# Attention and two gated layers on one core: SyncE asks for a batch's loads in another order

## Chip, core and metric

The kernel runs on one core of one Trainium2 chip. The metric is the device time of one execution in microseconds.

## What is computed

Eight batches of 8 heads, 576 positions and head size 64; all arithmetic is float32, and the large products are done in three float32r products each (high x high, high x low, low x high).

```python
def sm_attn(qq, kk, vv):
    s = scale * np.matmul(qq, kk.transpose(0, 1, 3, 2))
    a = np.exp(s - np.max(s, axis=-1, keepdims=True))
    a = a / (np.sum(a, axis=-1, keepdims=True) + 1e-09)
    return np.matmul(a, vv)
p_packed = sm_attn(p, k, v)                # 32 packed rows per head
x = sm_attn(q, p_packed, p_packed)         # -> 4608 tokens x 512
xn = x / rms(x) * rms_g
g = xn @ w_gate                            # 512 x 1536
y = (silu(g) * (xn @ w_val)) @ w_out       # 1536 x 512
h = ((y @ w1) * (y @ w2)) @ w3             # 512 x 1024, then 1024 x 1024
out = h @ w_out2                           # 1024 x 512
```

## The kernel before

**Stages.** (1) A fused product, `wf = w3 @ w_out2`, in eight row blocks (`fuse`, L668 to L670), with the attention of batch 0 threaded between its pieces. It ends 65 us into the span. (2) Eight batches of 24 slots each, some 88 us a batch. (3) The last layer, from about 770 us to the end, which the change does not touch.

**A slot.** Slot n (f = n // 2 within the batch, t = n % 2) computes 128 rows of gate and value for 288 tokens on TensorE (`into`, L688 to L690). ScalarE takes tanh (L1005), VectorE makes g_s and g_h (L1240, L1246), ScalarE casts the high half of g_hx (L1012), VectorE subtracts to get the low half (L1260). Two slots fill one g_hx tile k = n // 2 (there are two such tiles). From slot 2 on TensorE also does half of the output product of tile n // 2 - 1 (`outof`, L708 to L710), 512 of the 576 tokens. The other 64 tokens of a tile go to memory with a 64 KB store, `rest_scratch<-g_hx`, which ScalarE issues in the even slots for the tile before (L986); the stores count up two semaphores in turn, and the cast in an odd slot waits until the store of the tile two before has landed, since it overwrites that tile.

**Attention between the slots.** After some slots an item of the next batch's attention runs on TensorE (the table `SLOT_ITEM`): M (a piece of the folded input weights, L652, six pieces per batch), S1 (scores of keys, L603), AT (L608), PV (values, L615), PT, S2 (scores of queries, L626), Z (L636), SS (L640). M(b,2) and M(b,3) are in slots 1 and 2, AT of the next batch in 3 and 4, PV in 5, PT in 6, S2 in 7 and 10, Z in 11 and 14, M(b,4) and M(b,5) in 12 and 13, SS in 16, M(b+1,0) and M(b+1,1) in 18 and 20, S1 of batch b+2 in 22 and 23. Batch 0's attention and S1(1,0) run inside the fused product, S1(1,1) after slot 0.

**Loads.** SyncE issues nearly all transfers in one order, written by hand, and stands still at each semaphore wait in it. The loads: `load_kp(a)` packed queries and keys of batch a (L342, L343), waits for S1 of batch a - 1; `load_v(a)` values (L350), waits for PV(a - 1); `load_q(a, t)` half of the queries (L357), waits for S2(a - 1, t); `load_w_in(a, part)` a 1 MB piece of w_gate or w_val (L366, two buffers), waits for the M item two pieces before; `load_wo(i)` rows of the first w_out (L400), in four transfers of 0.25, 0.75, 1 and 1 MB. `spread_r(a)` stores the inverse norms and reads them back to all partitions (L371, L375), for GpSimd to scale a2T (L536); `store_wf(half)` stores a half of wf (L386), `store_y` the result of a batch (L380).

Of the kernel before, what the change touches and what calls it, by code (L numbers as in the profile page):

```python
# [116 lines left out]
def build(nc, kT_d, qT_d, v_d, pT_d, g_d, w_gate, w_val, w_o, w12, w3T, w_out, out, r_dram, y_dram, wf_dram, rest_dram):  # L117
    ctx = ExitStack()
    with ctx:
# [191 lines left out]
        def full(eng, kind, a, part):  # L311

            eng.wait_ge(xy_full, number[kind, a, part] + 1)
# [22 lines left out]
        def _(sp):  # L336
            def load_kp(a):
                if a >= B:
                    return
                if a > 0:  # L340
                    full(sp, "S1", a - 1, 1)
                sp.dma_start(pT[:], pT_d[a]).then_inc(p_loaded, 16)  # L342
                sp.dma_start(kT[:], kT_d[a]).then_inc(k_loaded, 16)  # L343

            def load_v(a):
                if a >= B:
                    return
                if a:
                    full(sp, "PV", a - 1, 0)
                sp.dma_start(v_sb[:], v_d[a]).then_inc(v_loaded, 16)  # L350

            def load_q(a, t):
                if a >= B:
                    return
                if a:
                    full(sp, "S2", a - 1, t)
                sp.dma_start(qT[t][:], qT_d[a, t]).then_inc(q_loaded[t], 16)  # L357

            def load_w_in(a, part):
                if a >= B:  # L360
                    return
                n = PIECES * a + part
                if n >= W_BUFS:
                    full(sp, "M", *divmod(n - W_BUFS, PIECES))
                group, which = divmod(part, 2)
                sp.dma_start(w_in[n % W_BUFS][:], (w_gate, w_val)[which].rearrange("(c p) n -> p c n", p=P)[:, :, BANK * group:BANK * (group + 1)]  # L366
                             ).then_inc(w_in_loaded[n % W_BUFS], 16)

            def spread_r(a):
                sp.wait_ge(rr_ready, a + 1)  # L370
                sp.dma_start(r_dram[:, S * a:S * (a + 1)].rearrange("o (p j) -> (o p) j", j=NT), rr[:]).then_inc(r_stored, 16)  # L371
                sp.wait_ge(r_stored, 16 * (a + 1))
                if a:
                    sp.wait_ge(a2s_ready, 2 * a)
                sp.dma_start(r_sb[:], r_dram[:, S * a:S * (a + 1)].to_broadcast([P, S])).then_inc(r_loaded, 16)  # L375

            def store_y(tile):
                sp.wait_ge(res_act, 2 * (tile + 1))
                sp.wait_ge(res_dve, 2 * (tile + 1))
                sp.dma_start(y_tiles[tile], g_res[:]).then_inc(y_stored, 16)  # L380

            def store_wf(half):
                sp.wait_ge(wf_act, 2 * (half + 1))
                sp.wait_ge(wf_dve, 2 * (half + 1))
                rows = slice(4 * half, 4 * half + 4)
                sp.dma_start(wf_v[:, rows, :], (wf_first, wf_second)[half][:]).then_inc(wf_stored[half], 16)  # L386
# [11 lines left out]
            def load_wo(i):  # L398
                rows = WO_LOADS[i]
                sp.dma_start(wo_raw[:, rows, :], wo_v[:, rows, :]).then_inc(wo_loaded[i], 16)  # L400
# [15 lines left out]
            for part in range(2):  # L416
                load_w_in(0, part)
            load_kp(1)
            store_wf(0)
            spread_r(0)  # L420

            sp.wait_ge(fuse_done, 2 * 4)
            load_wo(0)
            for part in range(2, 4):
                load_w_in(0, part)
            load_wo(1)
            store_wf(1)
            load_q(1, 0)
            sp.wait_ge(wf_stored[1], 16)
            load_wo(2)  # L430
            load_v(1)
            load_wo(3)
            load_q(1, 1)

            for b in range(B):
                load_w_in(b, 4)
                load_w_in(b, 5)
                if b > 0:
                    store_y(b - 1)
                if b < B - 1:  # L440
                    load_kp(b + 2)
                    load_v(b + 2)
                    load_q(b + 2, 0)
                    load_q(b + 2, 1)
                    load_w_in(b + 1, 0)
                    load_w_in(b + 1, 1)
                    spread_r(b + 1)
                    load_w_in(b + 1, 2)
                    load_w_in(b + 1, 3)
# [920 lines left out]
```

## Time and profile before

| what | value |
|---|---|
| median of 3 runs (lowest, highest) | 1370.83 us (1370.05, 1372.01) |
| profiled execution | 1372.39 us, its span 1370.6 us |
| TensorE busy | 1351.6 us, 99% |
| VectorE, ScalarE, GpSimd busy | 60%, 31%, 9% |
| queue of SyncE's and ScalarE's transfers | 30.4% and 2.1% of the DMA engines' span |
| chain that ended last | TensorE 94%, DMA 3%, VectorE 2% |
| read from and written to memory | 112.99 MB, 27.28 MB |

The chain that ended last is followed back from the last instruction. TensorE holds most of it; the DMA share is where TensorE's work stood behind a transfer. With a busy share this high, the times at which TensorE waits, and the clock it was granted, say more than the shares do. Times of rows are microseconds from the start of the span.

### The profile page before, as it was taken

The page shows a single profiled execution, that of the slowest core. Times are in us where ns is not written, and L with a number is a line of the kernel's source. Part 1 is how long each engine was busy: PE and PEld are TensorE (multiplying, and loading weights), DVE is VectorE, ACT ScalarE, POOL GpSimd, SP SyncE. Part 2 cuts the span into 40 slices and gives each one's busy share as a digit, 9 for nine tenths or more (in the row PEclk, how much of TensorE's full clock was granted, in tenths as well). Part 3 has the DMA queues.
Part 4 walks back from the last instruction along what each step waited for, and adds up shares of the span by engine and source line. Part 5 has one row for each costly group of instructions (what it writes and reads, how often), then busy time and mean ns, then how long its engine had stood idle before and what let it go on. Part 6 is the DMA issues. An engine that isn't in the chain of part 4 may idle for free.

```text
span 1370.6 us, 24236 instructions
## 1 busy us (share of the span) xinstructions
PE 1351.6 (99%) x9992; PEld 1164.6 (85%) x9992; DVE 827.8 (60%) x1488; ACT 424.9 (31%) x836; POOL 128.1 (9%) x117
## 2 busy tenths in 40 slices
PE   9989999999999999999999999999999999999998
PEld 6767788788887878878788899999999999999997
DVE  4647666665576665766664568655546564556554
ACT  4333433433434334343333333121212121112211
POOL 0200101001010010010100530110101010110100
PEclk9999999999999999999999999999999999999999
DMA  9394263443634545332344450202020120202001
GB/s 326 124 328 145 81 190 124 154 134 105 191 91 129 157 139 173 106 99 83 113 132 151 174 185 1 62 1 62 1 62 28 35 62 1 62 1 62 1 32 31
DMA packets 89870, 141.84 MB, mean 103 GB/s; under 512 B 30624, under 2 KB 40864, under 8 KB 87968
## 3 DMA queue, kind: packets, MB, share of 16 engines
q1 hardware_dynamic: 63648, 133.99, 30.4%
q10 hardware_dynamic: 26112, 6.30, 2.1%
q8 instruction: 79, 1.29, 0.4%
q14 instruction: 31, 0.25, 0.1%
HBM read 112.99 MB, written 27.28 MB: 102 GB/s over the span
## 4 chain that ended last, share of the span: by engine, by line
PE 94%; DMA 3%; DVE 2%; ACT 0%; issue 0%; SPq 0%; DVEq 0%; ACTq 0%
PE psum L769 9%; PE psum L768 9%; PE psum L767 9%; PE psum L688 8%; PE psum L689 7%; PE psum L690 7%; PE psum L708 6%; PE psum L710 6%; PE psum L709 6%; PE psum L789 5%; PE psum L790 5%; PE psum L791 5%; PE psum L652 3%; PE psum L636 1%; DMA rest_scratch<-g_hx 1%; DMA wf_scratch<-wf_second 1%
## 5 line engine op out<-in xcount | busy, mean ns | idle before, releaser
L769 PE MATMUL psum<-xo_hi,w_lo 128*128 128x256 f32 x1008 | 285.3, 283 | 0.0
L768 PE MATMUL psum<-xo_lo,w_hi 128*128 128x256 f32 x1008 | 285.2, 283 | 0.0
L767 PE MATMUL psum<-xo_hi,w_hi 128*128 128x256 f32 x1008 | 285.1, 283 | 0.0
L688 PE MATMUL psum<-a_hi,m_hi 128*128 128x288 f32 x768 | 239.9, 312 | 0.2 <-DVE g_s L1240 0.2
L689 PE MATMUL psum<-a_lo,m_hi 128*128 128x288 f32 x768 | 226.7, 295 | 0.0
L690 PE MATMUL psum<-a_hi,m_lo 128*128 128x288 f32 x768 | 226.1, 294 | 0.0
L767 PEld LDWEIGHTS psum<-xo_hi,w_hi 128*128 128x128 f32 x1008 | 193.4, 192 | 1.4
L768 PEld LDWEIGHTS psum<-xo_lo,w_hi 128*128 128x128 f32 x1008 | 193.4, 192 | 1.4
L769 PEld LDWEIGHTS psum<-xo_hi,w_lo 128*128 128x128 f32 x1008 | 193.4, 192 | 0.0
L688 PEld LDWEIGHTS psum<-a_hi,m_hi 128*128 128x128 f32 x768 | 144.4, 188 | 54.5 <-issue 48.0
L1240 DVE SCALAR_TENSOR_TENSOR g_s<-g_s,psum 128x288 f32<-128x288 f32 x192 | 86.3, 450 | 120.1 <-ACT g_s L1005 119.4
L708 PE MATMUL psum<-g_hx,wo_hi 128*128 128x512 f32 x384 | 151.1, 393 | 2.8 <-DVE g_hx L1260 2.8
L1012 ACT CAST g_hx<-g_h 128x288 fp32r<-128x288 f32 x192 | 83.1, 433 | 225.9 <-DVE g_h L1246 221.2
L710 PE MATMUL psum<-g_hx,wo_lo 128*128 128x512 f32 x384 | 151.8, 395 | 0.0
L709 PE MATMUL psum<-g_hx,wo_hi 128*128 128x512 f32 x384 | 151.6, 395 | 0.0
L689 PEld LDWEIGHTS psum<-a_lo,m_hi 128*128 128x128 f32 x768 | 144.5, 188 | 3.7
L690 PEld LDWEIGHTS psum<-a_hi,m_lo 128*128 128x128 f32 x768 | 144.2, 188 | 0.0
L1260 DVE TENSOR_TENSOR g_hx<-g_h,g_hx 128x288 fp32r<-128x288 f32 x192 | 89.1, 464 | 75.6 <-ACT g_hx L1012 75.6
L789 PE MATMUL psum<-wf_hi,hh 128*128 128x512 f32 x288 | 112.6, 391 | 0.5 <-DVE h_lo L1320 0.5
L790 PE MATMUL psum<-wf_lo,hh 128*128 128x512 f32 x288 | 112.5, 391 | 0.0
L791 PE MATMUL psum<-wf_hi,h_lo 128*128 128x512 f32 x288 | 112.0, 389 | 0.0
L1005 ACT ACTIVATE g_s<-psum 128x288 f32<-128x288 f32 x192 | 78.6, 410 | 106.7 <-PE psum L690 106.7
(144 smaller groups left out, 1883.2 us busy)
## 6 DMA issues: line engine op xcount, KB each, us to landing
w_in<-in_w_gate SPq DMA_DIRECT2D x24, 1024.0 KB, 5.3
w_in<-in_w_val SPq DMA_DIRECT2D x24, 1024.0 KB, 5.4
kT<-in_kT SPq DMA_DIRECT2D x8, 1152.0 KB, 11.1
v_sb<-in_v SPq DMA_DIRECT2D x8, 1152.0 KB, 7.5
qT<-in_qT SPq DMA_DIRECT2D x16, 576.0 KB, 4.4
y_scratch<-g_res SPq DMA_DIRECT2D x9, 1024.0 KB, 8.7
x<-y_scratch SPq DMA_DIRECT2D x32, 256.0 KB, 5.6
out<-b_res SPq DMA_DIRECT2D x8, 1024.0 KB, 5.4
```

The source lines that it names most:

```text
L688: nc.tensor.matmul(in_ps[which], hi, a2_hi[:, t, par, :], start=par == 0, stop=False)
L689: nc.tensor.matmul(in_ps[which], hi, a2_lo[:, t, par, :], start=False, stop=False)
L690: last = nc.tensor.matmul(in_ps[which], lo, a2_hi[:, t, par, :], start=False, stop=par == 1)
L708: nc.tensor.matmul(out_ps[m], hi, hh, start=f == 0, stop=False)
L709: nc.tensor.matmul(out_ps[m], hi, hl, start=False, stop=False)
L710: last = nc.tensor.matmul(out_ps[m], lo, hh, start=False, stop=f == FC - 1)
L767: nc.tensor.matmul(dst, hi, xo_hi[:, i, c, :], start=c == 0, stop=False)
L768: nc.tensor.matmul(dst, hi, xo_lo[:, i, c, :], start=False, stop=False)
L769: last = nc.tensor.matmul(dst, lo, xo_hi[:, i, c, :], start=False, stop=c == 1)
L789: nc.tensor.matmul(out2_ps[m], hh2[:, f, cols], wf_hi[:, chunk, :], start=(p, f) == (0, 1), stop=False)
L790: nc.tensor.matmul(out2_ps[m], hh2[:, f, cols], wf_lo[:, chunk, :], start=False, stop=False)
L791: last = nc.tensor.matmul(out2_ps[m], hl2[:, f, cols], wf_hi[:, chunk, :], start=False, stop=end)
```

## The change

It moves calls in SyncE's order and nothing else. Batch 1's values, pieces 2 and 3 of batch 0 and both halves of batch 1's queries are asked for before the fused product is done. In each batch's loop the loads of batch b + 2 stand behind pieces 0 and 1 of batch b + 1.

```diff
             load_kp(1)
+            load_v(1)
             store_wf(0)
+            load_w_in(0, 2)
             spread_r(0)
+            load_w_in(0, 3)
+            load_q(1, 0)
+            load_q(1, 1)
 
             sp.wait_ge(fuse_done, 2 * 4)
             load_wo(0)
-            for part in range(2, 4):
-                load_w_in(0, part)
             load_wo(1)
             store_wf(1)
-            load_q(1, 0)
             sp.wait_ge(wf_stored[1], 16)
             load_wo(2)
-            load_v(1)
             load_wo(3)
-            load_q(1, 1)
 
             for b in range(B):
                 load_w_in(b, 4)
                 load_w_in(b, 5)
                 if b > 0:
                     store_y(b - 1)
                 if b < B - 1:
+                    load_w_in(b + 1, 0)
+                    load_w_in(b + 1, 1)
                     load_kp(b + 2)
                     load_v(b + 2)
                     load_q(b + 2, 0)
                     load_q(b + 2, 1)
-                    load_w_in(b + 1, 0)
-                    load_w_in(b + 1, 1)
                     spread_r(b + 1)
                     load_w_in(b + 1, 2)
                     load_w_in(b + 1, 3)
```

On SyncE, around the end of the fused product, the order before was (v_sb and qT are batch 1's values and queries, the two w_in pieces 2 and 3 of batch 0, wo_raw the first w_out):

```order
L343 DMA kT<-in_kT 128x2304
L386 DMA wf_scratch<-wf_first 128x4x512
L371 DMA r_scratch<-rr 96x6
L375 DMA r_sb<-r_scratch 128x576
L400 DMA wo_raw<-in_w_o 128x512
L366 DMA w_in<-in_w_gate 128x4x512
L366 DMA w_in<-in_w_val 128x4x512
L400 DMA wo_raw<-in_w_o 128x3x512
L386 DMA wf_scratch<-wf_second 128x4x512
L357 DMA qT<-in_qT 128x1152
L400 DMA wo_raw<-in_w_o 128x4x512
L350 DMA v_sb<-in_v 96x3072
```

It is now:

```order
L343 DMA kT<-in_kT 128x2304
L350 DMA v_sb<-in_v 96x3072
L386 DMA wf_scratch<-wf_first 128x4x512
L366 DMA w_in<-in_w_gate 128x4x512
L371 DMA r_scratch<-rr 96x6
L375 DMA r_sb<-r_scratch 128x576
L366 DMA w_in<-in_w_val 128x4x512
L357 DMA qT<-in_qT 128x1152 x2
L400 DMA wo_raw<-in_w_o 128x512
L400 DMA wo_raw<-in_w_o 128x3x512
L386 DMA wf_scratch<-wf_second 128x4x512
L400 DMA wo_raw<-in_w_o 128x4x512 x2
```

Values, both pieces and the queries stand ahead of all of wo_raw; after it nothing but wf_second is left.

On SyncE, in the turn of one batch b (from 1 to 5), before and now; y_scratch is the result of batch b - 1, pT, kT, v_sb and qT belong to batch b + 2, r_scratch and r_sb to b + 1:

```order
 L380 DMA y_scratch<-g_res 128x4x512
+L366 DMA w_in<-in_w_gate 128x4x512
+L366 DMA w_in<-in_w_val 128x4x512
 L342 DMA pT<-in_pT 128x128
 L343 DMA kT<-in_kT 128x2304
 L350 DMA v_sb<-in_v 96x3072
 L357 DMA qT<-in_qT 128x1152 x2
-L366 DMA w_in<-in_w_gate 128x4x512
-L366 DMA w_in<-in_w_val 128x4x512
 L371 DMA r_scratch<-rr 96x6
 L375 DMA r_sb<-r_scratch 128x576
```

The two pieces of batch b + 1, which wait for M(b,4) and M(b,5) in slots 12 and 13, now stand ahead of the loads of batch b + 2. The orders of TensorE, VectorE, ScalarE and GpSimd are unchanged.

## Rows read from the trace of the kernel before

**Rows 1.** Waits of TensorE, 60 to 120 us: who, for whom, total us, times, longest

```profile
PE psum L615 <- DMA v_sb<-in_v: 3.4, 1, 3.4
PE psum L708 <- DVE g_hx L1260: 2.8, 1, 2.8
PE psum L652 <- DMA w_in<-in_w_gate: 2.2, 1, 2.2
```

**Rows 2.** Busy time by stretch: length, PE, PEld, DVE, ACT, POOL, clock, DMA, GB/s

```profile
65.40:116.70 51.30, 42.06 (x386) 33.56 (x380) 27.13 (x55) 19.88 (x43) 0.00 (x0) 0.93 0.85 276
253.00:293.50 40.50, 40.50 (x384) 33.19 (x376) 24.46 (x50) 17.18 (x37) 0.00 (x0) 1.00 0.53 162
```

**Rows 3.** Timeline of TensorE in batch 0: start, us, operation, idle before

```profile
67.15 0.71 PE L603 MATMUL psum<-kT,pT 64*32 64x288 f32 x16
...
92.18 2.79 PE L615 MATMUL psum<-v_sb,a1T 96*32 96x64 f32 x96 [3.39 <-DMA v_sb<-in_v]
...
113.14 0.80 PE L708 MATMUL psum<-g_hx,wo_hi 128*128 128x512 f32 x1 [2.76 <-DVE g_hx L1260]
```

**Rows 4.** Timeline of SyncE's issues after the fused product

```profile
65.20 0.43 SPq L366 DMA_DIRECT2D w_in<-in_w_gate  x1
...
81.11 0.50 SPq L350 DMA_DIRECT2D v_sb<-in_v  x1
```

**Rows 5.** Issues at 92.9, 95.0, 97.8, 102.7 us: KB, us to landing

```profile
kT<-in_kT SPq DMA_DIRECT2D x1, 1152.0 KB, 14.2
v_sb<-in_v SPq DMA_DIRECT2D x1, 1152.0 KB, 16.9
rest_scratch<-g_hx ACTq DMA_DIRECT2D x1, 64.0 KB, 14.3
qT<-in_qT SPq DMA_DIRECT2D x1, 576.0 KB, 10.5
```

**Rows 6.** Timeline of SyncE, two issues that follow each other in batch 1

```profile
217.47 0.38 SPq L366 DMA_DIRECT2D w_in<-in_w_val  x1
231.01 0.33 SPq L371 DMA_DIRECT2D r_scratch<-rr  x1
```

**Rows 7.** Issues at 176.56, 177.6, 182.1 and 217.5 us: KB, us to landing

```profile
y_scratch<-g_res SPq DMA_DIRECT2D x1, 1024.0 KB, 8.7
kT<-in_kT SPq DMA_DIRECT2D x1, 1152.0 KB, 10.7
rest_scratch<-g_hx ACTq DMA_DIRECT2D x1, 64.0 KB, 6.4
w_in<-in_w_val SPq DMA_DIRECT2D x1, 1024.0 KB, 5.2
```

**Rows 8.** Timeline of ScalarE (cast of g_hx) and of TensorE (slots 17, 18)

```profile
112.16 0.43 ACT L1012 CAST g_hx<-g_h 128x288 fp32r<-128x288 f32 x1 [4.65 <-DMA rest_scratch<-g_hx]
230.36 0.43 ACT L1012 CAST g_hx<-g_h 128x288 fp32r<-128x288 f32 x1 [1.01 <-DVE g_h L1246]
...
229.55 0.40 PE L708 MATMUL psum<-g_hx,wo_hi 128*128 128x512 f32 x1
...
230.92 0.29 PE L688 MATMUL psum<-a_hi,m_hi 128*128 128x288 f32 x1
...
232.51 0.40 PE L708 MATMUL psum<-g_hx,wo_hi 128*128 128x512 f32 x1
```

**Rows 9.** Busy time by stretch, columns as in rows 2; after two waits

```profile
72.00:74.00 2.00, 1.94 (x23) 1.13 (x24) 1.08 (x2) 0.75 (x1) 0.00 (x0) 1.00 1.01 296
114.00:116.00 2.00, 2.00 (x6) 1.07 (x5) 1.93 (x5) 0.43 (x1) 0.00 (x0) 0.50 0.00 0
```

**Rows 10.** Timeline of GpSimd and ScalarE: scaling and first reading of a2T

```profile
236.59 1.44 POOL L536 TENSOR_TENSOR a2T<-a2T,r_sb 128x576 f32<-128x576 f32 x1 [5.61 <-DMA r_sb<-r_scratch]
248.25 0.67 ACT L892 CAST a_hi<-a2T 128x576 fp32r<-128x576 f32 x1
```

**Rows 11.** An issue of ScalarE at 84.6 us: KB, us to landing

```profile
rest_scratch<-g_hx ACTq DMA_DIRECT2D x1, 64.0 KB, 8.8
```

## The prediction

> **What bounds the kernel now.** I read the page's busy shares first: TensorE is busy 99% of the span, so only its idle time and its half-speed time can move. The table of waits comes next. Between 60 and 120 us TensorE waits 3.4 us for the values of batch 1, 2.8 us for VectorE's low half of a g_hx tile and 2.2 us for input piece 2 [rows 1]; from 120 to 830 us, the other seven batches, the same view has no TensorE wait at all. So the change can win only in batch 0's first half.
>
> How much is lost there? Compare the 12 slots of batch 0 from 65.4 to 116.7 us with the same slots of batch 2: 51.3 us against 40.5, and the granted clock is 0.93 against 1.00 [rows 2]. Batch 0 has no output products in its first two slots, two times 1.4 us less work (a part starts at 229.55 and the next thing at 230.92 [rows 8]), and one extra S1 of 0.7 us [rows 3]. The loss is 10.8 + 2.8 - 0.7 = **12.9 us**: 8.4 are idle, in those three waits; most of the rest is work at 1.2 GHz after the two longer ones: the 96 small products that start at 92.18 take 2.79 us, and the product at 113.14 shows 0.80 us for 0.40 [rows 3, 8].
>
> Who is late? SyncE asks for everything in one order [rows 4]. Piece 2 was asked for at 65.20, as the fused product ended. The values of batch 1 stand behind a wait for the landing of wf_second and went out at 81.11. The third wait is a chain: ScalarE sat 4.65 us until 112.16 for a rest_scratch store, then cast g_hx, then VectorE subtracted, then TensorE went on at 113.14 [rows 3, 8]. That store of 64 KB was asked for at 97.8 and landed 14.3 us later, behind batch 2's keys (asked for at 92.9, 14.2 us) and values (95.0, 16.9 us) [rows 5]. Stores alternate between two semaphores, so the second half of product k needs store k - 2 landed, which was asked for three slots earlier.
>
> **The change, part by part.** *Batch 1's values, queries and pieces 2 and 3 amid the fused product.* Nothing is added, 4.3 MB change places. The rows ahead of them there stay early, and their own waits (PV, S2, M of batch 0) are met at about 25 to 56 us, so store_wf(0) and spread_r(0), which now have them ahead, are not held up; TensorE has no wait on a transfer in that stretch. The waits of 3.4 and 2.2 us go. The queue after 65 us keeps only wo_w, wf_second and pieces 4 and 5, so wo_w rows 1 to 3 also come sooner.
>
> *Batch 2's loads behind w_in(1,0) and w_in(1,1).* w_in(1,0) waits for M(0,4) of slot 12, so keys, values and queries are not asked for before slot 13. The stretch of 85 to 113 us, full of transfers today, becomes quiet and the third wait goes. I take **12.4 us** of the 12.9 off; 0.5 stays for slots 1 to 3, where VectorE still has shift1, two m_lo and the wo_lo split. Bounds: 8.4 (the three waits go, clock and rest stay) to 12.9.
>
> *The same move in every batch.* This part costs. Today batch 1's turn asks for w_in(2,1) at 217.47 and then nothing until 231.01 [rows 6], because keys, values and queries went out earlier, spread by their own waits. Now pT, kT, v and two qT follow at 217.9 to 220, since those waits have long been met: 3.5 MB in one burst. When does it end? w_in(2,1) lands at 217.47 + 5.2 = 222.7 [rows 6, 7]. pT and kT take 3.0 us (y landed at 176.56 + 8.7 = 185.3, kT at 177.6 + 10.7 = 188.3) [rows 7]. The values take 4.8 (from kT's landing at 107.1 to theirs at 111.9), one qT 1.3 (to 113.2) [rows 5]. Sum: 222.7 + 3.0 + 4.8 + 2.6 = 233.1.
>
> In that burst ScalarE issues the store of slot 14, at about 220.6, where today only w_in(2,1) is under way. A store issued while SyncE's transfers are under way lands with the last of those asked for before it: 182.1 + 6.4 = 188.5 beside kT's 188.3 [rows 7], and 97.8 + 14.3 = 112.1 beside the values' 111.9 [rows 5]. So the new landing lies between 230.5 (values done) plus the store's own second or so, and 235 (all done, with two stores). I take 233.9. Slot 17's cast needs it: it starts at 230.36 today [rows 8]. From landing to TensorE took 1.0 us (112.1 to 113.14) [rows 5, 3]: TensorE resumes at 234.9 instead of 232.51 [rows 8], a **new wait of 2.4 us** under the name "L708 <- DVE g_hx". Behind the waiting cast stand only ScalarE's next tanh and VectorE's next products, which TensorE needs a slot later. Ends: 0 (landing by 231.5) and 3.5 us (235).
>
> DMA: Bandwidth & Descriptors of the Trainium skill (Queues, rings and completion order) says that each DMA engine goes round-robin between the rings of SyncE and ScalarE, packet by packet, by which a small store need not sit out what was asked for before it; the same section says that the semaphore's increment lands after every earlier write of that engine. The rows side with the second half; by the first alone the new wait would be near nothing, a rival below.
>
> Then the clock. After the 2.2 us wait the granted clock stayed 1.00 (2.4 GHz), after the 2.8 us one it fell to 0.50 (1.2 GHz) [rows 1, 9]; there six matmuls took some 2.9 us in place of 1.4, a cost of 1.5 us. A wait of 2.4 lies between: half the times, 0.75 us on average. The burst occurs for b = 0 to 5 (batch b + 2 exists): 6 x (2.4 + 0.75) = **+18.9 us**; with the ends, 0 and 6 x (3.5 + 1.5) = +30.
>
> *Priced at nothing.* Keys now land at about 226 and S1 of that batch runs at slot 22, some 20 us later; values and queries are needed in the next batch. spread_r stands behind the burst: r_scratch goes out at 231.01 [rows 6] and may land at about 235, so r_sb and GpSimd's scaling move from 236.59 to some 240; two scalings end by 243, and ScalarE reads a2T at 248.25 [rows 10]. That cover is 5 us. In the first slots of a batch 2.4 MB fewer compete, where nothing waits.
>
> *Sum.* The profiled execution took 1372.39 us with a span of 1370.6; the median of the runs is 1370.83, so the span's differences are applied to the median: 1370.8 - 12.4 + 18.9 = 1377.3.
>
> **The rivals.** (A) *The stores come through and only the gain is left.* For it: round-robin between the rings, and a store at the height of batch 0's queue, asked for at 84.6, that took only 8.8 us [rows 11]. Against it: the two landings above. Price: landing by 231.5 gives 1370.8 - 12.4 = 1358.4; the side is decided at a cost of 2.1 us per batch, a landing of about 233.6 without loss of clock. Partly so, with 0.3 to 1.7 us each, gives 1360 to 1368. (B) *It cancels*: landings near 233.5, TensorE's clock held, within 0.2% of 1370.8. (C) *A new wait takes batch 0's place*: VectorE's load in slots 1 to 3, or the wo_w rows, keep 4 us; with the burst's cost that gives 1381. (D) *The burst reaches further*, r_sb late for the a2 split and the clock lost each time: 1370.8 - 12.4 + 30 = 1388. (E) The change does not do what it says: SyncE's order is the only thing moved and every wait in front of the moved rows is met early, so hardly.
>
> **How the numbers follow.** Measurements of this kernel can tell about 0.2%, 2.7 us, from no change. Chances: forecast with C and D, 0.55 (C 0.08, D 0.07 of it); B 0.12; A in full 0.15 and in part 0.18. Predicted time 1377. The range reaches to full A but for its last microsecond, and up to where most of D is left out: 1359.5 to 1385; the likeliest case's own range is 1373.5 to 1384. Faster 0.33, same 0.12, slower 0.55.
>
> **What would show it.** Right: no TensorE wait on v_sb or w_in; batch 0's first 12 slots about 38.5 us long; six waits "L708 <- DVE g_hx", each at slot 18, with ScalarE waiting for rest_scratch before slot 17's cast, and stores of slot 14 taking 12 to 14 us. Wrong: those stores land within 11 us of their issue (A), TensorE waits at other slots (D), or batch 0 keeps a wait of over 1 us (C).

## The result, and the profile after

| | before | changed |
|---|---|---|
| median | 1370.85 us (7 runs) | 1375.45 us (7 runs, 1374.39 to 1378.86) |
| ratio | | 1.0039, 95% interval 1.0027 to 1.0050 |
| span of the profiled execution | 1370.6 us | 1373.6 us |

The kernel became slower by 0.4%, where 1377 had been forecast. TensorE's waits, in the same view as [rows 1] but over the whole span (who, for whom, total us, times, longest):

```profile
PE psum L708 <- DVE g_hx L1260: 10.5, 7, 2.7
...
PE psum L652 <- DVE m_lo L1085: 0.3, 1, 0.3
```

The waits for v_sb and for w_in are gone. The wait for g_hx, 2.8 us once before, is now 10.5 us in seven pieces. ScalarE's waits for a store stand behind it, six of them, 24.4 us in total:

```profile
ACT g_hx L1012 <- DMA rest_scratch<-g_hx: 24.4, 6, 5.0
```

Busy time by stretch, columns as in [rows 2]: slots 0 to 10 of batch 0, its slots 11 to 23, batch 1 and batch 3 as wholes:

```profile
65.10:104.20 39.10, 38.59 (x387) 31.18 (x379) 26.32 (x54) 19.98 (x43) 0.00 (x0) 1.00 0.49 169
104.20:154.70 50.50, 48.33 (x352) 38.21 (x344) 35.36 (x66) 19.94 (x40) 6.54 (x7) 1.00 0.55 171
154.70:245.00 90.30, 88.76 (x727) 71.36 (x719) 56.12 (x108) 34.19 (x71) 6.76 (x7) 1.00 0.43 135
334.50:427.20 92.70, 90.03 (x727) 71.81 (x719) 55.51 (x108) 34.20 (x71) 6.55 (x7) 0.98 0.42 131
```

The first stretch took 51.3 us before [rows 2], now 39.1. A batch of the same kind took 88.2 to 88.5 us before; the table shows 90.3 and 92.7. SyncE's issues in batch 1, and what became of four transfers of that burst (asked for at 209.1, 209.6, 210.1 and 210.8; KB, us to landing):

```profile
207.66 0.37 SPq L366 DMA_DIRECT2D w_in<-in_w_val  x1
208.07 0.50 SPq L342 DMA_DIRECT2D pT<-in_pT  x1
208.61 0.43 SPq L343 DMA_DIRECT2D kT<-in_kT  x1
209.09 0.43 SPq L350 DMA_DIRECT2D v_sb<-in_v  x1
209.58 0.93 SPq L357 DMA_DIRECT2D qT<-in_qT  x2
221.19 0.33 SPq L371 DMA_DIRECT2D r_scratch<-rr  x1
```

```profile
v_sb<-in_v SPq DMA_DIRECT2D x1, 1152.0 KB, 12.9
qT<-in_qT SPq DMA_DIRECT2D x1, 576.0 KB, 13.9
qT<-in_qT SPq DMA_DIRECT2D x1, 576.0 KB, 15.5
rest_scratch<-g_hx ACTq DMA_DIRECT2D x1, 64.0 KB, 12.4
```

Five transfers follow w_in in 3 us where nothing followed before [rows 6], and the 64 KB store of slot 14 takes 12.4 us. In the six bursts it took 13.0, 12.4, 11.9, 13.6, 13.7 and 11.5 us, and TensorE then waited 2.0, 1.4, 1.0, 2.7, 2.7 and 0.6 us at slot 18; the seventh piece of the total is 0.2 us at another slot. In batch 3 the cast starts after 5.0 us of idle, TensorE follows 1.0 us later:

```profile
404.29 0.43 ACT L1012 CAST g_hx<-g_h 128x288 fp32r<-128x288 f32 x1 [5.01 <-DMA rest_scratch<-g_hx]
```

```profile
405.27 0.50 PE L708 MATMUL psum<-g_hx,wo_hi 128*128 128x512 f32 x1 [2.67 <-DVE g_hx L1260]
```

### The profile page after: what moved, and what is told of

The parts are those of the page before. It is cut to its first block, busy times and chain, and to the rows that moved or that the text cites. A ratio compares the mean times of both kernels' runs of the same rounds, so it can differ in the third digit from the quotient of the medians.

```text
span 1373.6 us, 24236 instructions
## 1 busy us (share of the span) xinstructions
PE 1352.7 (98%) x9992; PEld 1163.9 (85%) x9992; DVE 827.0 (60%) x1488; ACT 424.2 (31%) x836; POOL 128.9 (9%) x117
## 4 chain that ended last, share of the span: by engine, by line
PE 89%; DMA 6%; DVE 3%; ACT 1%; issue 1%; ACTq 0%; DVEq 0%
PE psum L769 9%; PE psum L768 9%; PE psum L767 9%; PE psum L688 7%; PE psum L689 6%; PE psum L690 6%; PE psum L708 6%; PE psum L710 6%; PE psum L709 6%; DMA rest_scratch<-g_hx 6%; PE psum L789 5%; PE psum L790 5%; PE psum L791 5%; PE psum L652 4%; PE psum L615 1%; PE psum L668 1%
## 5 line engine op out<-in xcount | busy, mean ns | idle before, releaser
L708 PE MATMUL psum<-g_hx,wo_hi 128*128 128x512 f32 x384 | 152.0, 396 | 10.6 <-DVE g_hx L1260 10.5
L791 PE MATMUL psum<-wf_hi,h_lo 128*128 128x512 f32 x288 | 112.1, 389 | 0.0
## 6 DMA issues: line engine op xcount, KB each, us to landing
v_sb<-in_v SPq DMA_DIRECT2D x8, 1152.0 KB, 12.7
```

The costliest lines, as they stand in the source:

```text
L708: nc.tensor.matmul(out_ps[m], hi, hh, start=f == 0, stop=False)
L791: last = nc.tensor.matmul(out2_ps[m], hl2[:, f, cols], wf_hi[:, chunk, :], start=False, stop=end)
```

## The experiments

Each is told with the median of its runs and its ratio to the kernel before on the same chip. The ratio of the change itself, repeated in the last experiment, was 1.0036 there.

### 1. The early asks alone

```diff
                 if b < B - 1:
-                    load_w_in(b + 1, 0)
-                    load_w_in(b + 1, 1)
                     load_kp(b + 2)
                     load_v(b + 2)
                     load_q(b + 2, 0)
                     load_q(b + 2, 1)
+                    load_w_in(b + 1, 0)
+                    load_w_in(b + 1, 1)
```

> Only the early asks are kept (values, queries, pieces 2 and 3 amid the fused product); the loop's order is that of before. Theory (the loss is the new wait on the slot-14 store behind a burst in each of six batches; the gain is batch 0's three waits): no TensorE wait at slot 18 in any batch, batches 1 to 5 at 88.2 to 88.5 us again. The waits on v_sb and w_in are gone. Open is the third wait of batch 0: batch 2's keys, values and queries go out at 75 to 100 us again, but without batch 1's loads ahead of them, so I expect a store there of 8 to 10 us and no wait, and 1358.5 to 1360 us in all. Rival (the gain needs both halves, since the third wait comes from batch 2's loads being early): a wait on g_hx of 1 to 3 us in batch 0 stays, 1361 to 1363. Rival (the loss is not in the loop's order): 1370 or more.

1360.3 us, 0.9925 (0.9908 to 0.9942). No wait at slot 18; batch 0 took 87.6 us and batches 1 to 5 took 88.2 to 88.5. In batch 0 no wait on g_hx remains, so the rival that wanted both halves for the gain falls: all of the gain is in the early asks. Clearing the queue of batch 1's loads was enough to let batch 2's through in time. What is left on TensorE in the eight batches is the wait on m_lo and some tenths more:

```profile
PE psum L652 <- DVE m_lo L1085: 0.6, 1, 0.6
PE psum L652 <- ACT sc L859: 0.3, 1, 0.3
PE psum L688 <- DVE g_s L1240: 0.2, 1, 0.2
```

### 2. The loop's order alone

The edit is the other half: the kernel before with the two `load_w_in(b + 1, ...)` ahead of `load_kp(b + 2)`.

> Only the loop's order is changed; the first part is that of before. Theory: the six waits at slot 18 stay (10 us idle and up to 3 of half clock or more, 15 in sum), the waits on w_in (2.2) and v_sb (3.4) of batch 0 stay since the pieces and values are still asked for after the fused product, and only the third wait of batch 0 (2.8 and 1.5 of clock) goes: 1370.8 - 4.3 + 15 = 1381.5, between 1378 and 1386. Rival (moving batch 2's loads down also frees the earlier transfers and the v_sb wait with them): 1375 to 1377.

1382.68 us, 1.0090 (1.0072 to 1.0108), inside the theory's range. The waits on transfers of batch 0 are as long as before, and the wait for g_hx has the size that it has in the change:

```profile
PE psum L708 <- DVE g_hx L1260: 10.0, 9, 3.1
PE psum L615 <- DMA v_sb<-in_v: 3.4, 1, 3.4
PE psum L652 <- DMA w_in<-in_w_gate: 2.3, 1, 2.3
```

Six of the nine waits for g_hx are at slot 18 (8.8 us), the others are small ones at slot 20. None is in the first half of batch 0: the third wait of the kernel before is gone here too, without the early asks, and slots 0 to 10 took 47.8 us instead of 51.3. Each half of the change ends that wait by itself.

The two halves are told apart by these two kernels: the early asks give some 10 us. The loop's order costs some 12 us by itself, where it also ends the third wait, and some 15 on top of the early asks.

### 3. Queries behind spread_r

```diff
                     load_kp(b + 2)
                     load_v(b + 2)
-                    load_q(b + 2, 0)
-                    load_q(b + 2, 1)
                     spread_r(b + 1)
+                    load_q(b + 2, 0)
+                    load_q(b + 2, 1)
```

> The change, but in the loop the two query loads stand behind spread_r(b + 1) instead of ahead of it: the burst at slot 13 is 2.6 us shorter (1.15 MB less) and the store of slot 14 has only packed queries, keys and values ahead of it. Theory: that store lands when the values do, 13.3 to 14.3 us after w_in(b + 1, 1) was asked for instead of 15 to 16.8, that is about 10 to 11 us after its own issue; TensorE needs it within 11, so the waits at slot 18 shrink from 0.6 to 2.7 us each to 0 to 0.7, the clock never falls, total 1359 to 1362. Rival (the store shares the engines packet by packet and its time hangs on the number of transfers in flight, not on the ones ahead): a third less delay, waits of about 1 us each, 1366. Rival (the wait does not come from the burst): no change from 1375.

1363.57 us, 0.9951 (0.9931 to 0.9970), above the theory's range of 1359 to 1362 and below the first rival's 1366; the profiled execution, with a span of 1359.4, was the fastest of the six. The stores of slot 14 took 10.3 to 10.5 us in five bursts and 11.7 in batch 3, the one batch with a wait:

```profile
PE psum L708 <- DVE g_hx L1260: 0.7, 1, 0.7
```

So the point from which a store costs TensorE time is about 11 us (11.7 less the wait of 0.7), and the wait does come from the burst. Whether the store waits for what was asked for before it or shares the engines with it, this run does not decide.

### 4. The new order in batch 0 alone

```diff
                 if b < B - 1:
-                    load_w_in(b + 1, 0)
-                    load_w_in(b + 1, 1)
+                    if b == 0:
+                        load_w_in(1, 0)
+                        load_w_in(1, 1)
+                        spread_r(1)
                     load_kp(b + 2)
...
                     load_q(b + 2, 1)
-                    spread_r(b + 1)
+                    if b > 0:
+                        load_w_in(b + 1, 0)
+                        load_w_in(b + 1, 1)
+                        spread_r(b + 1)
```

> Early asks kept; in the loop only batch 0 keeps its new order, and there keys, values and queries of batch 2 go even behind spread_r(1); batches 1 to 5 have the order of before. Theory: slot 18 of no batch waits, batch 0's first 12 slots are quiet; total 1358 to 1359.5, the best of the four or equal to the kernel with the early asks alone. In batch 0 the loads go out at about 132 us, keys are needed at slot 22 (about 147), some 7 us after their landing, so no new wait. Rival (keys come too late there): a wait on kT of 1 to 5 us once.

1361.42 us, 0.9934 (0.9918 to 0.9951), not told apart from experiment 1 and above the forecast by some 2 us. One wait of 0.4 us for g_hx came at slot 20 of batch 0, where the late loads then were; keys were in time. The quiet stretch in the first half of batch 0 gained 0.8 us over experiment 1 (slots 0 to 10 took 39.0 us against 39.8), and slots 18 to 23 lost 1.0 (22.9 against 21.9).

### 5. A longer burst

```diff
+                    if b + 2 < B:
+                        sp.dma_start(pad_dram[b], v_d[b]).then_inc(pad_stored, 16)
                     load_kp(b + 2)
```

> The change, with one more 1.15 MB transfer in each of the six bursts: the values of batch b copied from memory to a scratch tensor that nothing reads, asked for between w_in(b + 1, 1) and the packed queries. It is work added, nothing is left out. Theory: everything asked for before the store of slot 14 delays it, so the store lands 3 to 5 us later than in the change (16 to 18 us after its issue instead of 11.5 to 13.7), each wait at slot 18 grows by as much (to 4.5 to 7 us) and the clock falls nearly each time (1.5 to 3 us more): 1375.5 + 6 x (3 to 5 + 1 to 2), that is 1399 to 1417. Rival (ring by ring sharing: only the loads themselves would be later): 1375 to 1380.

1361.77 us, 0.9932 (0.9909 to 0.9955). **Both theories are wrong here**: with 1.15 MB more in each burst the kernel is faster than the change by 1%. The burst did get longer, yet the store of slot 14 took only 7.3 to 10.2 us. Two transfers of batch 1 (the values asked for at 208.94, the store at 209.81; KB, us to landing):

```profile
v_sb<-in_v SPq DMA_DIRECT2D x1, 1152.0 KB, 15.1
rest_scratch<-g_hx ACTq DMA_DIRECT2D x1, 64.0 KB, 7.3
```

The store landed at 217.1, while keys, values and the first query half, all asked for before it, landed at 218.8, 224.1 and 225.4. "A store lands with the last of those asked for before it", the step that carried my prediction, is not a rule. What happens instead, the packets show. Packets moved per queue (q1 is SyncE's, q10 ScalarE's; packets, MB, share of the 16 engines' time) in the change from 215.5 to 219 us, while the values were under way:

```profile
q1 hardware_dynamic: 67, 0.82, 96.8%
q10 hardware_dynamic: 69, 0.02, 3.3%
```

In the kernel with the longer burst from 214.5 to 216.5 us, during the keys:

```profile
q1 hardware_dynamic: 89, 0.82, 97.1%
q10 hardware_dynamic: 88, 0.02, 4.6%
```

In both stretches one packet of the store went for one packet of SyncE's queue. In the change the store of 256-byte packets stood opposite to the values: 0.82 MB in 67 packets, 12 KB each, 3.5 us for 69 of its 256 pieces. With the longer burst it stood opposite to pT and kT, with small packets first and 9 KB ones after. The copy ahead of them went in large pieces (16 packets for 0.59 MB from 211.5 to 213.5) and was through when the store's turns began, some 4 us after its issue:

```profile
q1 hardware_dynamic: 16, 0.59, 68.3%
```

In the six bursts of the change and the six of this kernel the first packet of the slot 14 stores came 3.8 to 4.1 us after the issue. The last came after 10.9 to 11.3 us in the change and after 6.5 to 8.5 here. So the new theory: the store starts about 4 us after its issue, then waits for one packet of SyncE's queue with each of its own; its time hangs on the size of those packets, not on all that was asked for before.

### 6. No stores in batches 0 to 5

```diff
-                if t == 1 and k >= 2:
-                    act.wait_ge(rest_stored[k % 2], 16 * (k // 2))
+                if t == 1 and k >= 74:
+                    act.wait_ge(rest_stored[k % 2], stored((k - 72) // 2))
...
                 b, f = divmod(k, FC)
+                if b < 6:
+                    return
```

`stored(j)` counts what the two transfers of batch 6 add to the semaphores.

> The change without ScalarE's rest_scratch stores in batches 0 to 5 and without the casts' waits for them. Left out: the last 64 tokens of batches 0 to 5 aren't kept; in batch 6 each store writes its tile into seven places instead of one (two transfers), so that the last layer reads and computes as much as before, on wrong numbers. The bursts at slot 13 stay as they are. Theory (the loss goes through the store alone): no wait at slot 18, batches 0 to 5 at 87.2 and 88.2 us, all like the kernel with the early asks alone: 1358 to 1361.5, if batch 6 does not suffer from its larger stores. Rival (the burst slows TensorE by itself, through memory or through r_sb coming late): waits or longer slots stay, 1363 to 1375.

1360.47 us, 0.9920 (0.9899 to 0.9940). The bursts are as before and TensorE does not wait once at slot 18. From the first slot of batch 0 to that of batch 7 it took 614.7 us, against 630.5 in the change. The loss of the change goes through the stores and the casts' waits for them; the burst by itself slows nothing that these runs can tell.

### 7. Only the values early

```diff
             load_kp(1)
+            load_v(1)
             store_wf(0)
...
             load_wo(2)
-            load_v(1)
             load_wo(3)
```

> The kernel before with one call moved: load_v(1) goes out right after load_kp(1), as in the change; all else is that of before. Theory: of batch 0's losses the wait on v_sb goes with its half-speed products (3.4 and 1.3), the wait of 2.2 on w_in stays, and the queue after 80 us is 1.15 MB shorter, by 4.8 us; but TensorE also reaches slot 9 some 5 us sooner, while batch 2's keys and values still stand behind the pieces 4 and 5. I expect the third wait to shrink but not to go: 1370.8 - 4.7 - (0 to 4.3), that is 1362 to 1366. Rival (the third wait just grows by what the second one loses): 1368 to 1371.

1366.90 us, 0.9967 (0.9951 to 0.9984), a little above the theory's range. The wait on v_sb went, w_in's stayed, and the third wait kept most of its size:

```profile
PE psum L708 <- DVE g_hx L1260: 2.4, 1, 2.4
PE psum L652 <- DMA w_in<-in_w_gate: 2.3, 1, 2.3
```

After the wait on w_in the clock fell here (0.50, that is 1.2 GHz, where the kernel before was granted 1.00 [rows 9]), a loss that the theory did not have. From 74 to 77 us, columns as in [rows 2]:

```profile
74.00:77.00 3.00, 3.00 (x13) 2.81 (x13) 2.04 (x3) 1.57 (x4) 0.00 (x0) 0.50 0.97 350
```

### 8. Only pieces 2 and 3 early

```diff
             store_wf(0)
+            load_w_in(0, 2)
             spread_r(0)
+            load_w_in(0, 3)
...
-            for part in range(2, 4):
-                load_w_in(0, part)
```

> The kernel before with only the pieces 2 and 3 of batch 0 asked for amid the fused product, as in the change; values, queries and the loop are those of before. Theory: the wait of 2.2 on w_in goes, wf_second lands some 5 us sooner (2 MB less ahead of it), so the values go out at about 75 instead of 81 us and land at about 86, when PV needs them at 86: the wait on v_sb shrinks from 3.4 to 0 to 1.5; the third wait lies after that and shrinks too: 1360.5 to 1365. Rival (the waits on values are due to their own place in the queue alone): 3.4 stays or grows, since TensorE comes sooner, 1368 to 1371.

1363.30 us, 0.9942 (0.9920 to 0.9964), in the theory's range. The waits on w_in and on v_sb are both gone: with 2 MB less ahead of it the store of wf_second landed sooner (at 74.2 us instead of 80.7), and the values behind it with it (85.1 instead of 92.0). Two calls moved bring most of what all the early asks bring; the wait on g_hx keeps 1.6 us in batch 0.

### 9. The values last in the burst

```diff
                     load_kp(b + 2)
-                    load_v(b + 2)
                     load_q(b + 2, 0)
                     load_q(b + 2, 1)
+                    load_v(b + 2)
```

> The change with the burst in another order: packed queries, keys, both query halves, and the values last, the same transfers and bytes. My first theory (the store lands after all that was asked for before it) is in doubt since a longer burst made the kernel faster: by it the store of slot 14 still has all ahead of it, lands 11.5 to 13.7 us after its issue and the six waits stay, 1374 to 1378. New theory (the store starts some 4 us after its issue and then moves one 256-byte packet for each packet of SyncE's ring on every DMA engine, so it hangs on how large the transfers are that stand opposite to it, the 12 KB rows of the values above all): the store now stands opposite to the query rows of 4.6 KB, of which there are 16 per engine, and lands 7 to 9.5 us after its issue; no wait at slot 18, 1359 to 1362. The store of slot 16 then meets the values and takes 7 to 9 us, in time.

1360.47 us, 0.9919 (0.9906 to 0.9931). One call moved by two places takes the change from 1.0036 to 0.9919, with the same bytes in the same burst. The stores of slot 14 took 7.5 to 9.4 us; none of them made TensorE wait at slot 18, and one wait of 0.4 us for g_hx is left, at slot 20 of batch 5. In batch 0 (values asked for at 120.8, store at 121.6; packets from 125.5 to 129 us):

```profile
v_sb<-in_v SPq DMA_DIRECT2D x1, 1152.0 KB, 14.2
...
rest_scratch<-g_hx ACTq DMA_DIRECT2D x1, 64.0 KB, 7.7
...
q1 hardware_dynamic: 313, 1.36, 94.3%
q10 hardware_dynamic: 271, 0.07, 8.5%
```

The store was done at 129.3, the values asked for before it at 135.0. In 3.5 us all but one of its packets went (256 pieces, and the 16 packets of 4 bytes that each transfer has at its end), against 313 of SyncE's queue with 4.3 KB each on average: more turns in the same time. This is the new theory's forecast, and the first theory's (1374 to 1378) is out.

The size of the packets opposite is not the whole of it. From 129.5 to 133 us the values moved alone, without a store beside them:

```profile
q1 hardware_dynamic: 67, 0.82, 97.3%
```

That is the same count as beside the store in the change: the store did not slow the values. Worked out from these rows (length times 16 engines times share, over packets), a 12 KB packet of the values took 0.81 us, a 9 KB packet of the keys in experiment 5 took 0.35 and one of the mix here, mostly 4.6 KB rows of the queries, 0.17. Per byte the values took 1.7 times as long as the others; why, no run here tells. So what a turn of the store costs is the time of the packet opposite, and the values' were the dearest.

### 10. Half of each store

```diff
-                nc.scalar.dma_start(rest_dram[f][:, :, REST * b:REST * (b + 1)], g_hx[f % 2][:, :, TILE2:S].bitcast(F32)).then_inc(rest_stored[k % 2], 16)
+                nc.scalar.dma_start(rest_dram[f][:, 0, REST * b:REST * (b + 1)], g_hx[f % 2][:, 0, TILE2:S].bitcast(F32)).then_inc(rest_stored[k % 2], 16)
```

> The change with stores of the high half alone (128 pieces of 256 bytes, 8 per DMA engine, instead of 256 and 16). Left out: the low half of the last 64 tokens of every batch; the last layer reads the high half twice in its place, in two transfers per row block. The burst is that of the change. New theory (one packet of the store per packet of SyncE's ring): 8 turns instead of 16 to 17, so the store is done with the values' six rows and two query rows, 9 to 10.5 us after its issue instead of 11.5 to 13.7, waits at slot 18 of 0 to 0.3 us, 1359 to 1362. First theory (all that was asked for before it lands first): the landing moves by some 0.3 us at most, waits of 0.5 to 2.7 stay, 1373 to 1377.

1362.68 us, 0.9932 (0.9919 to 0.9946). Of the six waits at slot 18 two are left, in batches 1 and 3, beside two at slot 20, each of 0.5 to 0.6 us:

```profile
PE psum L709 <- DVE g_hx L1261: 2.4, 4, 0.6
```

The direction is the new theory's, the size only in part: the stores landed after 10.3 to 11.6 us instead of 9 to 10.5, and the time is a little above the range. In batch 1 the store landed at 208.6 + 11.5 = 220.1 and the values at 219.9:

```profile
v_sb<-in_v SPq DMA_DIRECT2D x1, 1152.0 KB, 13.0
...
rest_scratch<-g_hx ACTq DMA_DIRECT2D x1, 32.0 KB, 11.5
```

The packets kept to the forecast: the last piece of each store went 9.0 to 10.2 us after the issue. In batch 1, 127 of the 128 pieces had gone by 217.9, and the last went at 218.87, the moment at which the last packet of the values ended. The landing follows 1.0 to 2.2 us behind the last piece, a part that the theory had left out. It is not the values' landing that a store has to wait for: in batch 1, as in [rows 5, 7], it landed 0.2 us behind the transfer beside it, but in batch 3 the store landed at 398.35 and the values at 399.81, 1.5 us behind it.

DMA: Bandwidth & Descriptors of the Trainium skill (Queues, rings and completion order) says that the increment of a semaphore lands after every earlier write of that engine, across its queues. The trace agrees in that each of these stores landed behind its own last packet; whether it waits there for a write of the other queue, no run here tells.

### 11. The change again

> The change itself, unedited, on the chip of the two others. Both theories: six waits at slot 18 of 0.5 to 3 us, stores of slot 14 of 11.5 to 14 us, 1374 to 1378.

1376.47 us, 1.0036 (1.0022 to 1.0050). Waits at slot 18 of 1.7, 1.3, 0.6, 3.2, 2.3 and 0.4 us, in the same pattern over the batches as in the first profile.

## Why the prediction was right, step by step

**Which side, and by how much.** Forecast +6.5 us on the median, measured +4.6; 1375.45 lies in the likeliest case's own range. Of rivals, (A) would have needed stores landing within 11 us; none of the six did. Of (C) only 0.3 us for m_lo was there. Of (D) the clock fell twice in six, a2T was scaled 7 us before ScalarE read it, and beside slot 18 TensorE waited once, 0.2 us at slot 20. (B), within 0.2% of the time before, lies outside the interval (1.0027 to 1.0050).

**The gain.** Forecast 12.4 us. From the first slot to slot 18 of batch 0 TensorE took 77.3 us before and 65.1 after: 12.2 us. All three waits went, the 0.7 us one too, and the clock stayed at 2.4 GHz. Two small errors cancel in it. The stretch that I compared is slots 0 to 10, eleven slots and not 12, and its undisturbed length is 39.0 us (experiments 4 to 6), so the loss was 12.3 us and not 12.9: batch 0 has some 1.4 us less work there than batch 2, where I had put 2.1. And next to nothing of the loss stayed (39.1 us in the change, with 0.3 for m_lo), where I had left 0.5; 38.5 us could not have been reached.

One attribution was too narrow. I put the third wait down to batch 2's loads being early, and its end to the move in the loop. That move alone does end it (experiment 2), but so do the early asks alone (experiment 1), and experiments 7 and 8 show it shrinking from 2.8 to 2.4 and 1.6 us as the queue ahead gets shorter: the cause was the backlog as a whole. On top of the early asks the loop's move bought nothing that counts (experiment 4).

**The cost.** Forecast 6 x (2.4 + 0.75) = 18.9 us, measured 15.8: from the first slot of batch 0 to that of batch 7 the change took 630.5 us and the kernel without the stores 614.7 (experiment 6). 10.3 of it is idle in the six waits. Batches 3 and 4, whose clock fell, each took 4.5 us more than undisturbed, which is 1.8 more than their wait of 2.7, together 3.6; the other four batches took 1.9 more than their waits. The waits alone would have given 1368.7 on the forecast's own sum, the edge of (A) in part; that the time came near 1377 is also due to the 5.5 us beside them. The place (slot 18), the name in the table, the engine in between and the number of times were as forecast. The wait term was mis-sized: 2.4 us was meant, 0.6 to 2.7, on average 1.7, was found. The landing at 13.3 us behind the issue was too late by 0.6 us, for stores took 11.5 to 13.7 (mean 12.7). The turns do not make that spread: in all six bursts the last packet of the store ended 10.9 to 11.4 us after the issue, and the landing followed 0.6 to 2.4 us later. What makes this last part long in some batches stays open.

**The step that was right by luck.** The size came from "a store lands with the last of those asked for before it". Experiments 5 and 9 break that sentence: 7.3 to 10.2 us with more ahead of it, 7.5 to 9.4 with the same ahead of it in another order. In the change the rule comes near the landing because two errors in it cancel. The burst took longer than my sum: in batch 1 its last transfer, the second query half, landed at 225.6, 14.8 us after the store's issue instead of 12.5. And the store landed 2.4 us ahead of that transfer, though the store was asked for behind it, since the store's turns ran from the values' first rows only into the queries. The third wait of the kernel before is the same case: that store's packets went from 101.7 to 109.9 us, beside keys and values, and it landed at 112.1 [rows 5].

The sentence from the Trainium skill that I set against the rule (DMA: Bandwidth & Descriptors, Queues, rings and completion order), round-robin between the rings packet by packet, is what the packet counts show: 69 against 67, 88 against 89. What I drew from it, "the new wait would be near nothing", did not follow: a turn costs the time of the packet opposite, and the values' packets make it dear.

**The clock.** I took the fall to 1.2 GHz for half of the waits, between one of 2.2 us without and one of 2.8 with it. It fell after the two waits of 2.7 and not after 2.0 or less: a third of the waits, at a cost of at most 0.6 us on average (3.6 over six) instead of 0.75.

## What to carry to other kernels

When loads are moved down a queue, ask what small transfer of another engine will run beside them, how many packets it has, and how long each packet opposite to it takes: here the order inside a burst (the values, with the slowest packets, last) was worth over 1%. Moves of the two kinds in one change should be timed apart; this one held a gain of some 10 us and a loss of some 15. The best versions found, the early asks alone (0.9925) and the whole change with the values last (0.9919), both beat the kernel before and the change, and their intervals overlap.

## What was not expected of the hardware

**A longer burst made the small store faster**: 7.3 us instead of 12.4 in batch 1, with 1.15 MB more asked for ahead of it (experiment 5). The added copy held back the values, so that the store's turns fell on the keys.

**The length of a wait does not decide whether the clock falls.** In experiment 2 TensorE waited 3.10 us in batch 3 and was granted 1.00 (2.4 GHz) in the stretches around it; in experiment 11 it waited 2.30 us in batch 4 and was granted 0.51 right after (1.2 GHz for nearly all of it). A wait of 2.3 us lost the clock in experiment 7 too, where one of 2.2 at the same place of the kernel before had not. In both of the first two it had worked without a break before. Stretches around the two waits, of experiment 2 and then of experiment 11:

```profile
408.00:411.00 3.00, 3.00 (x20) 2.72 (x19) 0.83 (x2) 0.00 (x0) 1.44 (x2) 1.00 0.97 284
411.00:414.00 3.00, 0.20 (x2) 0.00 (x0) 0.21 (x1) 0.68 (x2) 0.00 (x0) 1.00 0.44 151
414.00:417.00 3.00, 2.70 (x23) 1.32 (x23) 1.52 (x4) 0.50 (x2) 0.00 (x0) 1.00 0.18 53
```

```profile
491.00:494.00 3.00, 3.00 (x21) 2.76 (x20) 1.15 (x4) 0.33 (x1) 1.53 (x2) 1.00 0.97 295
494.00:497.00 3.00, 0.70 (x6) 0.46 (x5) 0.56 (x2) 0.74 (x2) 0.00 (x0) 1.00 0.50 180
497.00:500.00 3.00, 3.00 (x14) 1.93 (x22) 1.17 (x3) 0.43 (x1) 0.00 (x0) 0.51 0.32 87
```

Open is why the store starts some 4 us after its issue when SyncE's queue is full, where the first packet of an undisturbed one went after 1.2 us and the store had landed after 1.9; the runs did not try that.
